# A recurrence and two mixture-of-experts layers on one core: small VectorE steps on ScalarE, and another order of the prologue

## The reference

```python
# 1. recurrence: batch 4, 8 heads, 768 steps, head size 48
mag = sqrt(a_re**2 + a_im**2); scale = minimum(mag, 0.999) / (mag + 1e-6)
for t in range(768):                       # state S is complex, 48x48 per head
    S = a[t] * S (complex, per row) + k[t] v[t]^T (real part)
    y[t] = q[t] @ S_re
# 2. x is [3072, 384]
h = x @ w_in                               # [3072, 1024]
e = exp(h - max(h)); solu = h * e / (sum(e) + 1e-9)
ln = (solu - mean) / sqrt(var + 1e-6) * g_ln
x = ln @ w_out                             # [3072, 384]
# 3. noisy top-2 gate over 8 experts
logits = x @ w_gate + log1p(exp(x @ w_noise)) * noise
out[token] = sum over its top 2 experts: weight * (relu(x @ w1[e]) @ w2[e])
```

## Time and profile before

| what | value |
|---|---|
| median of 3 runs | 1196.01 us (1194.78 to 1197.55) |
| the profiled execution | 1196.79 us, span 1195.0 us |
| granted TensorE clock, mean | 0.949 |
| busy share: PE, DVE, ACT, POOL | 87%, 74%, 52%, 39% |
| phase one, until about 634 us | TensorE and VectorE by turns |
| phase two, 634 to 1195 us | TensorE |

### The profile page before, as it was taken

The page is one execution under the profiler, slowest core; times in us unless marked ns, Lnnn a source line. Parts: engine busy times, 40 slices in busy tenths (PEclk is TensorE's granted clock), DMA queues, the critical chain, the costliest instruction groups (busy, mean ns, idle before and its releaser), DMA issues.

```text
span 1195.0 us, 21893 instructions
## 1 busy us (share of the span) xinstructions
PE 1036.7 (87%) x7866; PEld 979.6 (82%) x7866; DVE 887.2 (74%) x1729; ACT 618.1 (52%) x967; POOL 468.4 (39%) x417
## 2 busy tenths in 40 slices
PE   0036898998898899989947999999999999999996
PEld 0035797897797798878847999999999999999996
DVE  6888989988989989845554776776767777677672
ACT  6354555754754745534533555555555555555551
POOL 4122232443543533344532434434543543453442
PEclk9987899898899899989977999999999999999998
DMA  9420130230130121211406676776667667676640
GB/s 255 154 78 21 44 104 27 58 96 28 55 100 27 47 55 38 58 34 54 126 15 212 215 252 227 247 241 231 248 225 263 248 217 248 216 253 221 218 152 1
DMA packets 85980, 167.51 MB, mean 140 GB/s; under 512 B 18566, under 2 KB 57696, under 8 KB 85872
## 3 DMA queue, kind: packets, MB, share of 16 engines
q1 hardware_dynamic: 72432, 137.71, 35.9%
q0 software_dynamic: 13440, 28.40, 6.5%
HBM read 148.83 MB, written 21.92 MB: 143 GB/s over the span
## 4 chain that ended last, share of the span: by engine, by line
PE 61%; DVE 3%; issue 2%; ACT 1%; DMA 1%; POOL 0%; POOLq 0%; another core or an unknown queue 0%; DVEq 0%; ACTq 0%; SPq 0%
PE bank L1387 22%; PE bank L1567 22%; PE bank L1431 4%; PE bank L1479 4%; PE bank L1378 3%; PE bank L1453 2%; PE bank L1491 1%; PE bank L1497 1%; PE bank L1511 1%; PE bank L1468 0%; DVE zl L1212 0%; DVE w1l L1098 0%; DVE turn L999 0%; DMA xg<-xs,mine 0%; PE bank L1407 0%
## 5 line engine op out<-in xcount | busy, mean ns | idle before, releaser
L911 ACT ACTIVATE hh<-bank 128x256 fp32r<-128x256 f32 x248 | 95.3, 384 | 255.8 <-PE bank L1387 254.8
L1387 PE MATMUL bank<-sxh,w1h 128*128 128x256 f32 x744 | 212.0, 285 | 2.1 <-DVE sxl L1337 2.1
L1387 PE MATMUL bank<-sxh,w1l 128*128 128x256 f32 x744 | 210.3, 283 | 0.0
L1387 PE MATMUL bank<-sxl,w1h 128*128 128x256 f32 x744 | 210.0, 282 | 0.0
L1356 DVE SCALAR_TENSOR_TENSOR hl<-bank,hh 128x256 fp32r<-128x256 f32 x248 | 104.8, 423 | 120.1 <-ACT hh L911 110.0
L681 POOL DMA_INDIRECT out<-yo,mine x62 | 78.0, 1259 | 276.8 <-DVE yo L1349 267.4
L1567 PE MATMUL bank<-w2h,hh 128*128 128x384 f32 x496 | 167.2, 337 | 0.0
L1567 PE MATMUL bank<-w2l,hh 128*128 128x384 f32 x496 | 166.6, 336 | 0.0
L1567 PE MATMUL bank<-w2h,hl 128*128 128x384 f32 x496 | 166.4, 335 | 0.0
L1387 PEld LDWEIGHTS bank<-sxh,w1h 128*128 128x128 f32 x744 | 140.6, 189 | 2.5 <-DVE sxl L1337 2.5
L1387 PEld LDWEIGHTS bank<-sxh,w1l 128*128 128x128 f32 x744 | 141.5, 190 | 0.0
(11 more groups left out here) (196 smaller groups left out, 2445.7 us busy)
## 6 DMA issues: line engine op xcount, KB each, us to landing
raw<-in_w SPq DMA_DIRECT2D x62, 1536.0 KB
ar<-in_a_re SPq DMA_DIRECT2D x6, 768.0 KB, 4.6
turn<-in_a_im SPq DMA_DIRECT2D x6, 768.0 KB, 6.3
qk<-in_q SPq DMA_DIRECT2D x48, 96.0 KB, 2.3
qk<-in_k SPq DMA_DIRECT2D x48, 96.0 KB, 2.4
out<-wide SPq DMA_DIRECT2D x9, 512.0 KB, 11.8
vt<-in_v SPq DMA_DIRECT2D x24, 192.0 KB, 2.6
xs<-x SPq DMA_DIRECT2D x24, 192.0 KB, 2.7
```

What stands on the lines that cost most here:

```text
L911: nc.scalar.activation(hh[:, f % NH, :], bank[:, f % 2, 0:CAP], ACT.Relu).then_inc(hh_done, 1)
L1387: ins = MM(dst, stationary[a_](cc), moving[b_](cc), start=(n_ == 0), stop=(n_ == len(terms) - 1))
```

## The change

The parts of the edit:

1. Four small steps per tile move from VectorE to ScalarE: the negated maximum, the sum plus 1e-9 (as an Identity with a bias from a third column of `tiny`), the mean, and the logits' copy, which now stands at the top of ScalarE's body. The first four tiles' state, which was zero plus the new term, is a copy on ScalarE; later tiles keep the add on VectorE.
2. The five copies of `products_start` become ScalarE's `first_entries`, after the negations.
3. Unit 1 (q = 2, 3): both additions are made by TensorE, as products with the identity matrix into PSUM banks 0 to 3, right after its constants are ready; ScalarE reads the sums from PSUM. ScalarE's logs and scale of unit 1, the eight scalings of the second weight matrix and its high part now stand before `inverse_squares` of unit 0.
4. VectorE's `norm(2)` and `norm(3)` stand behind `newton(1)`, ahead of the loop. The first spread of the inverses is issued half by SP and half by ScalarE. `products_start(1)` stands at the end of body 0.
5. In body n = 1 VectorE's fills of 3 and 10 products are left out, so that all 20 products follow the q products; GpSimd's m2 of unit 2 stands behind the mask, and ScalarE's first squares of unit 2 behind its state copy.

```diff
+        def summed(q):
+            return bank[:, 2 * (q % 2):2 * (q % 2) + 2, :].rearrange("p b x -> p (b x)")[:, 0:2 * NG * HALF * BI]
...
+        def spread_first(eng, h_):
+            t = rcs[0].rearrange("p n h c x i -> p n (h c x i)")
+            for from_, to, g in SPARE[NG * h_:NG * (h_ + 1)]:
+                eng.dma_start(t[to, NG], t[from_, g]).then_inc(rc_spread, 16)
...
@@ SyncE
             spread_cum(0)
-            spread_rc(0)
+            sp.wait_ge(rc_done, 2)
+            spread_first(sp, 0)
@@ GpSimd
-            pool.wait_ge(cum_step, CUM)
-            for q in (2, 3):
-                m2(q)
-            for q in (2, 3):
-                zsum(q)
...
-                if b == 1 and c + 2 < C:
+                if b == 1 and 0 < c < C - 2:
                     m2(2 * c + 4)
...
+                if c == 0 and b == 1:
+                    m2(2 * c + 4)
                 if b == 1 and c + 2 < C:
                     zsum(2 * c + 4)
@@ ScalarE, prologue
             for q in (0, 1):
                 neg(q)
+            first_entries(0)
             act.wait_ge(raw_loaded, 48)
             nc.scalar.activation(wi_hi[0:PR], raw_in[0:PR], ACT.Copy).then_inc(w_hi_ready, 1)
             for q in (2, 3):
                 squares(q)
+            for q in (2, 3):
+                logs(q)
+            for q in (2, 3):
+                scale(q)
+            act.wait_ge(small_loaded, 64)
+            for c_ in range(FC):
+                nc.scalar.activation(raw_out[:, c_, :], raw_out[:, c_, :], ACT.Copy, scale=g_sb[:, c_:c_ + 1]).then_inc(w_scaled, 1)
+            act.wait_ge(w_scaled, FC)
+            nc.scalar.activation(wo_hi[:], raw_out[:], ACT.Copy).then_inc(w_hi_ready, 1)
             for q in (0, 1):
                 inverse_squares(q)
             for q in (0, 1):
                 inverse(q)
+            act.wait_ge(rc_done, 2)
+            spread_first(nc.scalar, 1)
             for q in (2, 3):
-                logs(q)
-            for q in (2, 3):
-                scale(q)
-            act.wait_ge(w_scaled, FC)
-            nc.scalar.activation(wo_hi[:], raw_out[:], ACT.Copy).then_inc(w_hi_ready, 1)
+                neg(q)
+            first_entries(1)
@@ ScalarE, body of a tile
+                if has(g_):
+                    act.wait_ge(lg_mm, g_ + 1)
...
+                    nc.scalar.activation(lg[:, B - count + g_ - first], bank[:, 6, DM:DM + 2 * E], ACT.Copy).then_inc(lg_copy, 1)
...
+                if 0 <= m < B:
+                    act.wait_ge(w_mm, m + 1)
+                    act.wait_ge(zero_ready, 4)
+                    nc.scalar.activation(state[:, m].rearrange("p s n e -> p (s n e)"), bank[:, 6, 0:2 * NP * D],
+                                         ACT.Copy).then_inc(w_added, 1)
...
                 if has(i):
+                    act.wait_ge(max_step, 2 * i + 1)
+                    nc.scalar.activation(nmax[:, 1:2], nmax[:, 0:1], ACT.Copy, scale=-1.0).then_inc(max_step, 1)
                     act.wait_ge(max_step, 2 * i + 2)
...
+                    act.wait_ge(exp_done, i + 1)
+                    wait(act, solu_step, 4 * i)
+                    nc.scalar.activation(esum[:, 1:2], esum[:, 0:1], ACT.Identity, bias=tiny[:, 2:3]).then_inc(solu_step, 1)
...
+                    act.wait_ge(solu_step, 4 * i + 3)
+                    nc.scalar.activation(mv[i % 2][:, 1:2], mv[i % 2][:, 0:1], ACT.Copy, scale=-1.0 / F).then_inc(solu_step, 1)
                     act.wait_ge(solu_step, 4 * i + 4)
                     nc.scalar.activation(z[:], z[:], ACT.Identity, bias=mv[i % 2][:, 1:2]).then_inc(centred, 1)
@@ VectorE
             newton(0)
             newton(1)
+            norm(2)
+            norm(3)
...
-                if first_one:
-                    products_start(c + 1)
...
-                fill(3)
+                if not first_one:
+                    fill(3)
...
-                if 0 <= m < LIVE:
+                if B <= m < LIVE:
...
-                fill(10)
+                if not first_one:
+                    fill(10)
...
                 if n == 0:
-                    weights_scaled()
                     weights_rest(0)
                     weights_rest(1)
+                    products_start(1)
@@ TensorE, ahead of the loop
+            def part_sum(q, sem_):
+                for first, count in ((0, 4), (4, 2)):
+                    cut = slice(first, first + count)
+                    for s_ in range(2):
+                        ins = MM(summed(q)[:, first * HALF * BI:(first + count) * HALF * BI], ident[:], mag(q, s_)[:, cut, :],
+                                 start=(s_ == 0), stop=(s_ == 1))
+                ins.then_inc(sem_, 1)
+            for q in (2, 3):
+                pe.wait_ge(sq_done, 2 * (q + 1))
+                part_sum(q, m2_done)
+            for q in (2, 3):
+                pe.wait_ge(ln_done, 4 * (q + 1))
+                part_sum(q, z_sum)
+            pe.wait_ge(sc_done, 4)
```

More of the change, by code:

```diff
@@ L326, in cum_part, with lines, cum_lines @@
             return cums[q // 2 % 2][:, s_, 0:NG, :, q % 2, :, :].rearrange("p g h x i -> p (g h) (x i)")
+        def lines(t):
+            return t.rearrange("p g h c (u v) i -> p (g h c u) v i", v=LINE)
+        def cum_lines(u):
+            return cums[u % 2][:, :, 0:NG].rearrange("p s g h c (u v) i -> p s (g h c u) v i", v=LINE)
         def mag(q, s_):
@@ L726, in scale @@
                 act.wait_ge(z_sum, q + 1)
-                nc.scalar.activation(f0, f0, ACT.Exp, scale=-1.0).then_inc(sc_done, 1)
+                nc.scalar.activation(f0, summed(q).rearrange("p (g x) -> p g x", x=HALF * BI) if 2 <= q < 4 else f0, ACT.Exp, scale=-1.0).then_inc(sc_done, 1)
             def neg(q):
@@ L732, in neg, with first_entries @@
                 nc.scalar.activation(part(an, q), part(ais[q // 2 % 2], q), ACT.Copy, scale=-1.0).then_inc(neg_done, 1)
+            def first_entries(u):
+                act.wait_ge(neg_done, 2 * (u + 1))
+                act.wait_ge(an_done, 6 * (u + 1))
+                wait(act, qp_done, 2 * B * (u - 1))
+                wait(act, kp_done, 2 * B * (u - 1))
+                wait(act, m_step, ENDS * (u - 1))
+                wait(act, cum_step, CUM * u)
+                ar, ai, cum = ars[u % 2], ais[u % 2], cum_lines(u)
+                for i, t in enumerate((ar, an, ai)):
+                    nc.scalar.activation(a0[:, i], t[:, :, 0, :, 0, :], ACT.Copy).then_inc(cum_step, 1)
+                nc.scalar.activation(cum[:, 0, :, 0], lines(ar)[:, :, 0], ACT.Copy).then_inc(cum_step, 1)
+                nc.scalar.activation(cum[:, 1, :, 0], lines(ai)[:, :, 0], ACT.Copy).then_inc(cum_step, 1)
             def inverse_squares(q):
@@ L798, in body @@
                 ahead = c + 2 < C
-                starting = prep and b == (1 if c == 0 else 0)
+                first_one = c == 0 and b == 1
+                starting = 0 < c < C - 1 and b == 0
+                if has(g_):
+                    act.wait_ge(lg_mm, g_ + 1)
+                    group, first, count = GROUP_ENDING[min(t for t in GROUP_ENDING if t >= g_)]
+                    wait(act, sp_done, 2 * group)
+                    wait(act, gate_step, gated(group))
+                    nc.scalar.activation(lg[:, B - count + g_ - first], bank[:, 6, DM:DM + 2 * E], ACT.Copy).then_inc(lg_copy, 1)
                 if n > T:
@@ L835, in body @@
                     neg(2 * c + 3)
-                if b == 1 and ahead:
+                    first_entries(c + 1)
+                if b == 1 and ahead and c > 0:
                     squares(2 * c + 4)
@@ L929, in _ @@
             V.memset(tiny[:, 1:2], -LN_LIMIT).then_inc(tiny_ready, 1)
+            V.memset(tiny[:, 2:3], 1e-9).then_inc(tiny_ready, 1)
             V.memset(state[:], 0.0).then_inc(zero_ready, 1)
@@ L932, in _ @@
             V.memset(wide[:], 0.0).then_inc(zero_ready, 1)
[L934 to L938, removed]
             def weights_rest(part):
@@ L1198, in gate @@
                         V.tensor_tensor(picked[:, from_:B], hot[:, from_:, 0], hot[:, from_:, 1], ALU.add).then_inc(gate_step, 1)
-                if has(g_):
-                    dve.wait_ge(lg_mm, g_ + 1)
-                    group, first, count = GROUP_ENDING[min(t for t in GROUP_ENDING if t >= g_)]
-                    wait(dve, sp_done, 2 * group)
-                    wait(dve, gate_step, gated(group))
-                    V.tensor_copy(lg[:, B - count + g_ - first], bank[:, 6, DM:DM + 2 * E]).then_inc(lg_copy, 1)
                 if n > T:
@@ L1226, in body @@
                     positions(g_ - 1)
-                if first_one:
-                    norm(2 * c + 2)
-                    norm(2 * c + 3)
                 if b == 0 and 0 < c < C - 1:
@@ L1254, in body @@
                     par = i % 2
-                    dve.wait_ge(exp_done, i + 1)
-                    V.tensor_scalar(esum[:, 1:2], esum[:, 0:1], 1e-9, None, ALU.add).then_inc(solu_step, 1)
-                    fill()
```

(6 more changed lines are left out.)

21 lines of the change are left out of this document (5 added, 16 removed).

## The result

The changed kernel takes 1190.24 us (median of 15 runs, 1180.77 to 1193.09); the kernel before took 1194.78 us on the same chip (15 runs, 1191.93 to 1197.63). The ratio is 0.995, interval 0.9934 to 0.9966: 6.0 us faster by the ratio (4.1 to 7.9), 4.5 by the two medians.

What follows compares the result with a forecast made beforehand. Bounds: a serial chain for 83 us, then VectorE in most tiles of chunks 0 to 4, TensorE in the others, last chunk and expert phase. Terms −8.5 − 2.7 + 1.5 = −9.7 gave 1186.5 us, range 1181.5 to 1192.5.

Steps and rivals of the forecast that it cites:

- ScalarE before the inverse: Prologue: sums, logs, scalings and wo_hi queued on ScalarE start the first inverse squares at 52.3 instead of 48.98, +3.3 us.
- Inverse, spread, weigh: Prologue: inverse −0.4, done at 60.8; spread's hole −1.45, weigh at 64.5; weigh 0.42 instead of 1.79 us, −1.35.
- Scalings off VectorE: Tile 0: eight weight scalings leave VectorE, −2.65 us; the weight remainders stay and end at 75.4.
- Tile 1: Second tile: VectorE idles about 5.5 us for xh, xl follows at 83.0; tile 2 begins at 92.4, −5.5 us so far.
- Tiles 2 and 3: Rest of chunk 0: waits, state adds and small steps save 2.2 us in tile 2, 0.8 in tile 3; −8.5 by chunk's end.
- Steady tiles: VectorE-bound tiles: small steps leaving VectorE save 0.3 us per tile in 9 tiles, −2.7 us.
- Rival C: Small steps save nothing, returning as waits for ScalarE; +3 us in the TensorE-bound tiles: 1190.5, chance 0.1.
- TensorE-bound tiles and tail: 12 TensorE-bound tiles and serial tail: ScalarE's two steps add 0.1 to 0.27 us, +1.5 us; bounds 0 and +4.
- Rival A: Prologue sums on TensorE stay at the half clock; inverse squares start at about 57.5, +5.2 us: 1191.7, chance 0.15.
- Rival B: Prologue: ScalarE ready in time, inverse starts at 49.5 to 50; half-clock stretches may go: 1182.5, chance 0.14.
- Rival D: Every tile: ScalarE's added steps stand serially, 0.6 us each in 24 tiles, +14, slower than before: 1201.5, chance 0.05.
- Rival E: Prologue gives nothing: the hole stays as long and xh's wait eats the rest: 1194, chance 0.06.

Runs made afterwards that it cites:

- second group: Prologue reorderings of the changed kernel; the one meant moves xh of tile 0 ahead of ScalarE's four logs of unit 2: 1187.14 us, ratio 0.9947.
- small steps alone: The kernel before with only the small steps, state copy and first entries of units 2 to 5 on ScalarE, old prologue: 1194.37 us, ratio 1.0006.
- prologue alone: The changed kernel with small steps, state copy and first entries of units 2 to 5 back on VectorE: 1189.27 us, ratio 0.9958.
- all three: The changed kernel with weights behind the spread, xh ahead of logs, x2 ahead of inverse squares: 1178.52 us, 0.9877; with small steps back on VectorE 1177.57, 0.9871.
- second profile: Profile from measuring the changed kernel again, unaltered: span 1190.9 us; that measurement's median 1190.52 us, ratio 0.9964.
- weights late: The changed kernel with eight weight scalings and wo_hi moved from ahead of the inverse to behind ScalarE's three spread DMAs: 1186.29 us, ratio 0.9933.
- the first experiment: The changed kernel measured again, unaltered: 1190.52 us (1181.26 to 1196.69), ratio 0.9964 against the kernel before.
- x2 first: The changed kernel with x2 ahead of the inverse squares and scale in chunks 0 to 4: 1183.99 us, ratio 0.9925; two further kernels add both prologue edits.

## Why the forecast came out as it did

The forecast was 1186.5, the median 1190.24: inside the range, faster as forecast, 3.7 us above the likeliest value. The prologue's mechanism was right in nearly every step; the gain in the steady tiles was not there. By its steps:

*ScalarE before the inverse, +3.3:* +3.0 (51.99 for 52.3). The two first sums took 7.95 us together: 5.3 + 2.7 = 8.0 had been taken for one at half clock and one at full. Later sums took 2.85, not 2.7. The eight scalings took 4.15, not 3.7: 0.52 us apart, where the row of ScalarE gave 0.46. That row was an operation of the same size that reads a bank; these read SBUF. Whether this makes the difference was not tried. The Trainium skill (ScalarE: Activation LUTs, What ACT_TABLE_LOAD costs) would have given 0.51 for it; the trace agrees with the page and not with my row. The excess of 0.5 us was covered by a chain of sums and logs that began 0.9 us sooner than I had it (29.24, not 30.1).

*Inverse, spread, weigh:* 60.4 for 60.8; 64.06 for 64.5; 0.43 for 0.42. *Scalings off VectorE:* remainders end at 75.0 for 75.4. These stand.

*Tile 1:* xl at 82.96 for 83.0, but for another reason in part. The idle time was 3.5 us and not 5.5, since kp took 3.62 us instead of 1.29 beside GpSimd's m2 of 2.23. I had priced that contention for qp (1.92 for 1.28) and missed it for kp. It cost nothing, since VectorE would have waited for xh anyway; with xh early it stands on the path (second group: xl begins only when kp ends). By the rule of the Trainium skill (SBUF — State Buffer, Who interferes with whom) the two exclude each other, and the trace agrees: 2.33 us longer beside an operation of 2.23.

*Tiles 2 and 3, −8.5 at the end of chunk 0:* tile 2 began at 92.31 for 92.4, thus −5.6 as forecast. Then the first reduce came at 97.26 and not at 96: the wait of 0.45 us for TensorE was gone, but one product beside GpSimd's mask took 1.13 us instead of 0.36, which I had left out:

```profile
95.24 1.23 POOL L632 TENSOR_SCALAR_AFFINE_SELECT at<-at 128x1024 f32<-128x1024 f32 x1 [10.91 <-ACT at L890]
95.56 1.13 DVE L1019 TENSOR_TENSOR ct<-cum,ar 128x192 f32<-128x192 f32 x1
```

The reduces of tiles 0 to 3 came 5.4, 7.3, 7.2 and 6.5 us earlier, that of tile 4 6.8, thus 1.7 less than forecast. What took the rest is open. TensorE's half clock may have a part in it (between reduces 0 and 4 the mean granted clock was 0.85, before 0.91), but from 79 to 147 us it was 0.75 in both.

*Steady tiles, −2.7: this is the step that failed.* It measured 0 within the noise in four comparisons (small steps alone 1.0006; prologue alone 0.9958 against 0.9964; all three 0.9877 against 0.9871; the gain between reduces 4 and 17 between 6.2 and 7.0, without a trend); 1 to 3 us at reduces 18 and 19 stay open. I read "busy 22.0 of 23.0 us" as bound by VectorE, so that each microsecond off it would count. But of its 37.7 idle us in 400, 16.4 were already waits for ScalarE (11.4, 3.5 and 1.5). VectorE and ScalarE wait for each other in turn; taking work from one lets it arrive early where it waits for the other. Rival C had named this mechanism. Its 1190.5 is where the median lies, though partly by chance: its +3 us in the TensorE-bound tiles was not there (next paragraph), and the prologue gave less than its −8.5.

*TensorE-bound tiles and tail, +1.5:* in the last chunk, reduces 19 to 23 took 72.6 us before and 72.7 after, thus nothing. From the last reduce to the end before took 597.0 us, the changed kernel 597.8, its second profile 599.5. Among all profiles it was 597.4 to 599.5 with small steps on ScalarE and 597.0 to 598.9 with them on VectorE: not resolved.

With the first profile's terms the sum is −6.8 + 0 + 0.8 = −6.0, as the ratio has it, and this too is partly luck: it leaves out the 3.7 us at reduces 18 and 19, and the second profile of the same kernel has −4.7 at reduce 4 and 2.5 us in the tail. The first profile's −9.7 equals the forecast's sum, but by those 3.7 us and not by the steps that I summed. Rival A was wrong (one slow sum, not four). Rival B was wrong for this kernel, since the inverse started at 51.99; another order could reach it (weights late: 49.24). Rival D was wrong: the gain did not shrink from chunk to chunk (6.8 at reduce 4, 6.8 at 17; in the second profile 4.7 and 4.0, and 6.5 at the last). Rival E was wrong: the first reduce came 5.4 us earlier.

What bounds the last body of a chunk instead, as far as shown: the path reduce, exponential, ScalarE's four inverse squares and scale, x2, TensorE. Shortening it in five chunks gave 6.5 us by the medians, 4.7 by the ratios. What sets the other three tiles of a chunk was not isolated.

## What to carry to other kernels

An engine that is busy 95% of a stretch isn't yet the bound if the rest is waits for its partner: look at what it waits for and ask whether that partner would be sooner too. Before an order list grows on a lightly used engine, look at what stands last in it that someone waits for: three times here a long list stood ahead of a short step on the path. The change put one there (weights ahead of the inverse). Another had stood there before and came onto the path when the change took VectorE's filling products away (logs ahead of xh). The third stood there before as well (inverse squares ahead of x2). Moving these three took the ratio from 0.995 to 0.9877, some 9 us, more than the whole change gave. Where run-to-run spread is as large as the effect, compare the start of the same step from tile to tile, not spans, and in more than one profile: the two profiles of the changed kernel agreed to 0.4 us up to the third reduce and were 3.9 apart at the last.

## What the runs showed of the hardware

- A 128x768 fp32 add of two SBUF operands on GpSimd (1.9 to 2.2 us) stretched the VectorE operation beside it by most of its own length or all of it: products to between 1.85 and 1.97 us from 0.36, the pair kp from 1.29 to 3.62.
- Adding two 128x768 operands on TensorE by plain fp32 products with the identity (8 instructions, four of 512 and four of 256 columns) took 2.85 us each once TensorE had run; the first two together took 7.95, so the first about 5.1 by subtraction; and VectorE's products beside it kept their 0.35 us.
- Six small DMAs issued by one sequencer took 3.72 us, by two in parallel 1.83 and 2.12.
- Later in the changed kernel, six such DMAs were issued in 3.75 us; the VectorE step that waits for them started 1.5 us after the last issue in one execution and 3.2 us in another.
- The place and length of half-clock stretches (3.4 to 13.7 us each between the first and the last reduce) differ between two profiles of the changed kernel, whose runs spread over 12 us. From reduce 4 to 17 nine of the thirteen profiles took 285.5 to 286.3 us, all at a mean granted clock of 0.93. Of the other four, three were shorter at a higher clock (277.9 at 0.96, 278.1 at 0.95, 281.2 at 0.94) and one was not (286.6 at 0.95, all three reorderings). In the twelve runs of the first experiment the two shortest (1181.26, 1182.19) had a mean clock of 0.947 and 0.948, the others 0.936 to 0.941. That the one causes the other was not shown. The three kernels with x2 first spread over 6, 8 and 2 us, in 6, 5 and 4 runs.
